# Side jobs of 18 attention slots dealt out anew between GpSimd, ScalarE, VectorE and TensorE

## The reference

```python
scores = q @ k.T / 8; mask: 0 <= i - j < 64; attn = softmax(scores) @ v
x = attn as (2304, 512)
xn = x / sqrt(mean(x * x) + 1e-6) * rms_g          # by token
x = (silu(xn @ w_gate) * (xn @ w_val)) @ w_out     # d_ff 1536
out = (relu(x @ w_in) ** 2) @ w_out2               # d_ff 2048
```

## Time and profile before

| | |
|---|---|
| median of 3 runs | 885.33 us (883.21 to 885.65) |
| the profiled execution | 885.68 us, span 884.0 us |
| TensorE busy | 858.6 us, 97% |
| VectorE busy | 548.2 us, 62% |
| ScalarE busy | 472.3 us, 53% |
| GpSimd busy | 543.9 us, 62% |
| mean granted TensorE clock | 0.994 |

### The profile page before, as it was taken

One profiled execution on the slowest core, in us unless ns is written; L12 is line 12 of the kernel. 1 busy time (PEld: TensorE's weight loads), 2 busy tenths in 40 slices (PEclk: granted clock), 3 DMA queues, 4 the chain that ended last, 5 costly groups with the idle time before them and its releaser, 6 DMA issues.

```text
span 884.0 us, 16543 instructions
## 1 busy us (share of the span) xinstructions
PE 858.6 (97%) x6388; PEld 846.9 (96%) x6388; DVE 548.2 (62%) x617; ACT 472.3 (53%) x1000; POOL 543.9 (62%) x517
## 2 busy tenths in 40 slices
PE   6787999999999999999999999999999999999998
PEld 5676999999999999999999999999999999999998
DVE  4767766558658548755556777676477675577222
ACT  5996565645565635455555455444455443555332
POOL 3664488674589755378857468563386744585332
PEclk9998999999999999999999999999999999999999
DMA  7863122212222212222212222222422221421222
GB/s 239 282 222 100 42 72 73 66 49 65 86 72 73 63 52 70 70 80 73 73 54 68 76 66 73 66 60 61 150 70 77 61 61 60 150 74 29 54 67 96
DMA packets 87007, 75.01 MB, mean 85 GB/s; under 512 B 5520, under 2 KB 70032, under 8 KB 86928
## 3 DMA queue, kind: packets, MB, share of 16 engines
q1 hardware_dynamic: 86784, 73.65, 27.9%
q10 hardware_dynamic: 144, 0.29, 0.1%
HBM read 69.21 MB, written 4.72 MB: 84 GB/s over the span
## 4 chain that ended last, share of the span: by engine, by line
PE 93%; ACT 2%; DVE 2%; DMA 1%; issue 1%; POOL 1%; SPq 0%; DVEq 0%; POOLq 0%
PE banks L703 30%; PE banks L705 30%; PE banks L704 30%; ACT probs L976 2%; PE banks L613 1%; PE banks L669 1%; DMA q_sb<-in_qT 1%; DVE probsT L1224 1%; PE banks L684 0%; PE banks L677 0%; PE banks L643 0%; POOL sq L507 0%; DVE neg_max L1211 0%; DVE banks L1204 0%; DVE acts L1164 0%
## 5 line engine op out<-in xcount | busy, mean ns | idle before, releaser
L703 PE MATMUL banks<-xc_hi,w_hi 128*128 128x384 f32 x844 | 282.5, 335 | 0.2 <-DVE xc_lo L1196 0.2
L705 PE MATMUL banks<-xc_hi,w_lo 128*128 128x384 f32 x844 | 281.9, 334 | 0.0
L704 PE MATMUL banks<-xc_lo,w_hi 128*128 128x384 f32 x844 | 281.9, 334 | 0.0
L564 POOL TENSOR_TENSOR d_lo<-d_raw,d_hi 128x512 fp32r<-128x512 f32 x84 | 127.3, 1516 | 174.4 <-ACT d_hi L899 174.4
L703 PE MATMUL banks<-hs_hi,d_hi 128*128 128x384 f32 x672 | 225.1, 335 | 0.1
L705 PE MATMUL banks<-hs_hi,d_lo 128*128 128x384 f32 x672 | 224.5, 334 | 0.0
L704 PE MATMUL banks<-hs_lo,d_hi 128*128 128x384 f32 x672 | 224.5, 334 | 0.0
L1302 DVE TENSOR_TENSOR hs_lo<-h,hs_hi 128x768 fp32r<-128x768 f32 x84 | 86.4, 1029 | 137.1 <-ACT hs_hi L899 136.9
L703 PEld LDWEIGHTS banks<-xc_hi,w_hi 128*128 128x128 f32 x844 | 158.5, 188 | 0.5 <-DVE xc_lo L1196 0.5
L704 PEld LDWEIGHTS banks<-xc_lo,w_hi 128*128 128x128 f32 x844 | 158.5, 188 | 0.0
L705 PEld LDWEIGHTS banks<-xc_hi,w_lo 128*128 128x128 f32 x844 | 158.4, 188 | 0.0
(11 more groups left out here) (87 smaller groups left out, 1072.9 us busy)
## 6 DMA issues: line engine op xcount, KB each, us to landing
d_raw<-in_w_down SPq DMA_DIRECT2D x48, 256.0 KB, 2.6
w_raw<-in_w_gate SPq DMA_DIRECT2D x36, 256.0 KB, 2.9
w_raw<-in_w_val SPq DMA_DIRECT2D x72, 128.0 KB, 2.8
d_raw<-in_w_out SPq DMA_DIRECT2D x36, 256.0 KB, 2.6
v_sb<-in_v_rows SPq DMA_DIRECT2D x16, 384.0 KB, 3.8
w_raw<-in_w_in SPq DMA_DIRECT2D x24, 256.0 KB, 2.7
w_raw<-in_w_in SPq DMA_DIRECT2D x48, 128.0 KB, 2.6
q_sb<-in_qT SPq DMA_DIRECT2D x16, 288.0 KB, 4.8
```

The lines of the kernel that those rows point to most:

```text
L564: nc.gpsimd.tensor_tensor(d_lo[m % 2][:], d_raw[m % 2][:], d_hi[m % 2][:].bitcast(F32), ALU.subtract).then_inc(dlo_done, 1)
L703: pe.matmul(ps, w_h, v_h, start=first, stop=False, skip_group_check=joined)
L704: pe.matmul(ps, w_h, v_l, start=False, stop=False, skip_group_check=joined)
L705: return pe.matmul(ps, w_l, v_h, start=False, stop=last, skip_group_check=joined)
```

## The change

Round 0 gets its squares in part from GpSimd: all four of the first half (slots 8 and 9), two of four of the second (slot 11; the other two stay on ScalarE). GpSimd no longer sums the four pieces: PE does, with `first_sums`, 12 one-column products that add up in PSUM after slot 10, and 12 more after slot 12. The high parts of the first two weight tiles go from ScalarE to GpSimd (slots 5, 7 and 10), the second tile's low parts from slots 7 and 8 to 14 and 15. Root, inverse, diagonals, both spreads, normalisations and high and low parts of the tokens come one slot earlier, and the second spread goes into bank 5, after slot 16, where it waits for the normalisations of the first half. The plain products of the first tile begin in slot 17. v has four buffers, and its loads are issued behind those of k and q. Six products of the identity with itself come ahead of the first scores.

```diff
--- before.py
+++ after.py
@@
-VR = 3
+VR = 4
+WARM = 6
@@ sync: the loads of the attention stage
             for i in range(SEQS):
-                if i + 1 < SEQS:
-                    load_v(i + 1)
                 if i + QR < SEQS:
                     load_k(i + QR)
                     load_q(i + QR)
+                if i + 1 < SEQS:
+                    load_v(i + 1)
@@ gpsimd
-            def add_squares(c, k):
...
+            def high1_plain(u):
+                pool.wait_ge(w_raw_in[u], 32)
+                nc.gpsimd.tensor_copy(w_hi[u][:, 0:3 * HALF_K], raw_part(u, RAW_A21, 3)).then_inc(hi1_done, 1)
+
+            def high2_plain(u):
+                pool.wait_ge(w_a22_in[u], 16)
+                nc.gpsimd.tensor_copy(w_hi[u][:, P_A22 * HALF_K:(P_A22 + 1) * HALF_K],
+                                      raw_part(u, RAW_A22)).then_inc(hi2_done, 1)
+
+            def square_half(k, c):
+                of = half_cols(0, k, c)
+                nc.gpsimd.tensor_tensor(squares[0][k][:, c * NT:(c + 1) * NT], of, of, ALU.mult).then_inc(sq_pool, 1)
@@ gpsimd, after the scaling of slot g
-                if g in (5, 7):
-                    low1_plain((g - 5) // 2)
-                if g in (6, 8):
-                    low2_plain((g - 6) // 2)
-                if g in (9, 10, 11):
-                    add_squares(0, g - 8)
-                if g == 12:
-                    for k in (1, 2, 3):
-                        add_squares(1, k)
+                if g == 5:
+                    high1_plain(0)
+                if g == 6:
+                    low1_plain(0)
+                if g == 7:
+                    high2_plain(0)
+                    low2_plain(0)
+                if g in (8, 9):
+                    pool.wait_ge(o_out, O_DONE[A_GROUP + 1])
+                    for k in (2 * (g - 8), 2 * (g - 8) + 1):
+                        square_half(k, 0)
+                if g == 10:
+                    high1_plain(1)
+                    high2_plain(1)
+                if g == 11:
+                    pool.wait_ge(o_out, O_DONE[B_GROUP + 1])
+                    square_half(0, 1)
+                    square_half(1, 1)
+                if g == 13:
+                    diagonals(0)
                 if g == 14:
-                    diagonals(0)
+                    low1_plain(1)
+                if g == 15:
+                    low2_plain(1)
@@ tensor, slot 0
                         pe.wait_ge(consts, 6)
+                        for n in range(WARM):
+                            pe.matmul(bank[5][:, 0:P], ident[:], ident[:], start=True, stop=True)
                         pe.wait_ge(first_in, 32)
@@ tensor
+            def first_sums(c, ps):
+
+                for n in range(c * TB // 2, (c + 1) * TB // 2):
+                    for k in range(KT):
+                        mm = pe.matmul(ps[:, n:n + 1], squares[0][k][:, n * P:(n + 1) * P], ones[:, 0:1],
+                                       start=k == 0, stop=k == KT - 1)
+                if c == 1:
+                    mm.then_inc(ms_mm, 1)
@@ tensor, the slots
             for g in range(TAIL):
-                if g == 17:
-                    pe.wait_ge(exp_done, 17)
-                    spread_half(1, bank[1])
                 slot(g)
-                if g == 13:
-                    token_sums(0, bank[5])
-                if g == 15:
-                    spread_half(0, bank[5])
-                if g == 18:
+                if g == 10:
+                    pe.wait_ge(consts, CONSTS)
+                    pe.wait_ge(sq_pool, KT)
+                    first_sums(0, bank[5])
+                if g == 12:
+                    pe.wait_ge(sq_pool, KT + 2)
+                    pe.wait_ge(sq_done, 2)
+                    first_sums(1, bank[5])
+                if g == 14:
+                    spread_half(0, bank[5])
+                if g == 16:
+                    pe.wait_ge(norm_done, KT)
+                    spread_half(1, bank[5])
+                if g == 17:
+                    pe.wait_ge(exp_done, 17)
                     pe.wait_ge(lo1_done, 1)
                     plain(0, "ga", P_A11, "B11")
...
@@ scalar, the slots
-                if g in (4, 6):
-                    high1((g - 4) // 2)
-                if g in (5, 7):
-                    high2((g - 5) // 2)
-                if g == A_GROUP + O_LAG:
-                    act.wait_ge(o_out, O_DONE[A_GROUP + 1])
-                if 0 <= g - A_GROUP - O_LAG < KT:
-                    square_half(g - A_GROUP - O_LAG, 0)
                 if g == B_GROUP + O_LAG:
                     act.wait_ge(o_out, O_DONE[B_GROUP + 1])
-                    for k in range(KT):
-                        square_half(k, 1)
-                if g == 13:
+                    square_half(2, 1)
+                    square_half(3, 1)
+                if g == 12:
                     root(0)
-                if g in (16, 17):
-                    x_high(0, ("B11", "B21")[g - 16], KT)
-                if g in (18, 19):
-                    x_high(0, ("B12", "B22")[g - 18], 2 * KT)
+                if g in (15, 16):
+                    x_high(0, ("B11", "B21")[g - 15], KT)
+                if g in (17, 18):
+                    x_high(0, ("B12", "B22")[g - 17], 2 * KT)
```

More of the change, by code:

```diff
@@ L671, in token_sums @@
             def token_sums(q, ps):
-                pe.wait_ge(sq_sum, 3 * q + 6)
-                if q == 0:
-                    pe.wait_ge(consts, CONSTS)
+                pe.wait_ge(sq_sum, 3 * q)
                 for n in range(TB):
-                    mm = pe.matmul(ps[:, n:n + 1], diag[min(q, 1)][:, n * P:(n + 1) * P], ones[:, 0:1],
+                    mm = pe.matmul(ps[:, n:n + 1], diag[1][:, n * P:(n + 1) * P], ones[:, 0:1],
                                    start=True, stop=True)
                 mm.then_inc(ms_mm, 1)
+            def first_sums(c, ps):
[5 more added lines that the diff above has]
+                    mm.then_inc(ms_mm, 1)
             def spread_part(q, ps, n):
@@ L743, in _ @@
                     plain(0, "vb", P_A21, "B12")
+                if g == 20:
                     pe.wait_ge(x_split, split_count(0, "B22"))
@@ L901, in high1 @@
             def high1(u):
-                if u < PLAIN:
-                    act.wait_ge(w_raw_in[u % 2], 32)
-                    copy(w_hi[u % 2][:, 0:3 * HALF_K], raw_part(u, RAW_A21, 3), hi1_done)
-                    return
                 act.wait_ge(s_add, 4 * steps_done(u - 1) + 3)
@@ L915, in high2 @@
             def high2(u):
-                if u < PLAIN:
-                    act.wait_ge(w_a22_in[u % 2], 16)
-                    copy(w_hi[u % 2][:, P_A22 * HALF_K:(P_A22 + 1) * HALF_K], raw_part(u, RAW_A22), hi2_done)
-                    return
                 act.wait_ge(s_add, 4 * steps_done(u))
@@ L1228, in _ @@
                         ALU.mult).then_inc(pt_out, 1)
+                if g == 12:
+                    mean_square(0, bank[5])
                 if g == 13:
-                    mean_square(0, bank[5])
-                if g == 14:
                     inverse(0)
-                if g in (15, 16):
-                    if g == 15:
+                if g in (14, 15):
+                    if g == 14:
                         dve.wait_ge(rb_first, 1)
                         dve.wait_ge(gain_in, 16)
-                    for k in (2 * (g - 15), 2 * (g - 15) + 1):
+                    for k in (2 * (g - 14), 2 * (g - 14) + 1):
                         normalise(half_cols(0, k, 0), k, bank[5][:, 0:NT])
-                if g in (17, 18):
-                    if g == 17:
+                if g in (16, 17):
+                    if g == 16:
                         x_low(0, "B11")
                         dve.wait_ge(rb_first, 2)
-                    for k in (2 * (g - 17), 2 * (g - 17) + 1):
-                        normalise(half_cols(0, k, 1), k, bank[1][:, 0:NT])
+                    for k in (2 * (g - 16), 2 * (g - 16) + 1):
+                        normalise(half_cols(0, k, 1), k, bank[5][:, 0:NT])
+                if g == 17:
+                    x_low(0, "B21")
                 if g == 18:
-                    x_low(0, "B21")
-                if g == 19:
                     x_low(0, "B12")
                     x_sum(0, "T3")
-                if g == 20:
+                if g == 19:
                     x_low(0, "B22")
```

18 lines of the change are left out of this document (6 added, 12 removed).

## The result

| | before | after |
|---|---|---|
| median | 885.40 us (882.53 to 887.25, 20 runs) | 882.87 us (879.40 to 885.08, 20 runs) |
| the profiled execution | 885.68 us, span 884.0 | 882.57 us, span 880.8 |
| mean granted TensorE clock | 0.994 | 0.994 |

The ratio is 0.9973, with a 95% interval of 0.9961 to 0.9984: faster by 2.5 us. I had forecast 5.2: the time lies in the range, but only half of the gain came.

The account below looks back on a forecast made before the run. TensorE works unbroken from 85.59 us, so only reaching that stretch earlier counts. Stretch gains 0.4 + 1.25 - 0.5 - 0.45 + 3.9 + 1.55 = 6.15, less 0.95 for stalls, leave 5.2 us: 880.1 us, range 876.8 to 884.5.

Parts of the forecast that it names:

- Slots 12 to 16: Stretch between exponentials of slots 12 and 16: 16.69 us before, 17.15 after, a loss of 0.45, sums mostly hidden.
- Rival 3: Lower clock comes in slots 13 to 16, one slot of it costing 2.7 us: 882.8 us, chance 0.08.
- slots 0 to 5: Stretch from slot 0 to 5: 18.06 us before, 17.65 after, as a weight's high part leaves ScalarE; gain 0.4.
- the tail: After slot 17, to PE's full stretch: 6.81 us before, 5.25 after, with work moved one slot ahead; gain 1.55.
- the 0.95 us set aside for stalls: Subtracted from the summed gain of 6.15 us for PE stalls on nothing visible, expected to return in part.
- Slots 10 to 12: Stretch with PE's first block of sums, 2.9 us: 8.47 us before, 9.0 after, a loss of 0.5.
- rival 2: PE's sums take a full record each, 6.0 us in place of 2.9: 884.1 us, chance 0.13.
- Slots 5 to 10: Waits for q and k vanish, loop and GpSimd work come next: 18.27 us before, 17.0 after; gain 1.25.
- Slot 16 to 17: Second spread no longer waits for slot 16's exponentials: 8.40 us before, about 4.5 after; gain 3.9.
- Squares and casts: On GpSimd in slots 5 to 11: 1.0 us per 128x384 square, 0.9 per 128x768 cast.
- Rival 1: GpSimd becomes the bound in slots 5 to 14, its work meeting the doubled rate: 890.6 us, chance 0.07.
- Rival 4: Clock rises earlier: 0.9 us in the first scores, 0.3 in slots 1 to 3; 878.9 us, chance 0.12.

Follow-up runs that it names:

- run with 64 columns: Changed kernel with each of TensorE's sums of squares 64 columns wide in place of one: 881.56 us, ratio 0.9973.
- table early: Changed kernel with one small exponential right behind the root, so the table load doesn't wait for the output copy: 882.73 us, ratio 0.9968.
- the run with 64 columns alone: Kernel before with only the second spread moved and the sums on PE, these 64 columns wide in place of one: 882.29 us, ratio 0.9975.

## Why the prediction was off

**What bounds the kernel: right.** The stretch behind the slots is filled as before (796.95 of 799.99 us busy), and the result is found ahead of it.

**The failed step is "Slots 12 to 16", in the words "all but that lies beside slot 12 or below the table loads. Periods of 6.3 and 3.3".** The 6.3 was 9.02. I had followed two paths, scores to exponentials and root to table load, and let the sums hide below the second. The path that ends last is a third: sums, scores, value product, ScalarE's copy of the outputs, table load, exponentials. The load is not cover for PE's work but stands behind it, as ScalarE makes its copy first. From the rows, at full clock and with 2.9 us of sums, this chain would come to some 6.9 us: 0.6 more than forecast. It is an estimate: sums end near 56.4, scores 1.1, value product 1.2, copy 0.7, load 1.3. The run with 64 columns agrees (8.06 less its stall of 1.18 is 6.9), and the one profile at full clock in which the sums began earlier took 6.33, the 6.3 of the forecast. So the order of ScalarE is worth 0 to 0.6 us, and the other 2.1 us are the lower clock from 55.4 us on, in the sums, the scores and the value product. The sum of the prediction has PE at full clock there and puts nothing for it. The runs bear out the two together (both removed: period 5.98, time 2.3 to 2.8 us lower) and the chain (table early: the copy no longer ahead of the load). The split between clock and order rests on rows, and on one soft comparison across sessions.

**The rival of the lower clock came nearest, in part by luck.** Rival 3 had it in slots 13 to 16 for one slot and gave 882.8 us, with a chance of 0.08. That this is the measured 882.87 almost to the digit is luck: it charges 2.7 us for the clock where the rows give 2.1, and the rest is the chain and the 0.8 us of slots 0 to 5, less what the tail gained beyond its forecast and the 0.95 us set aside for stalls. Its reason did not hold either: a clock that falls after PE has stood waiting. Here PE had waited only 0.78 us (and 0.79 in the run with 64 columns, where the clock stayed up); what PE was doing when the clock fell were one-column products, which the earlier trace rows and the profile of before (low clock from 58.7 to 62.1 us, right behind `token_sums`) already showed once. I made four times as many of these products and did not ask what they had done to the clock. The Trainium skill, TensorE: Matmul & The Clock Gate, Part 1, which I had cited for the warm-up, says that activity brings the clock up. The trace agrees in so far as the six products had it up by slot 0 or 1 in five of eight profiles and in none without them; the sums show a second side, a PE that is busy in the records and yet loses its clock.

**The first part of the sums, "Slots 10 to 12", was right:** 9.06 against 9.0, block 2.74 against 2.9 (so rival 2, at 6.0, falls). In three other profiles the clock fell there as well, with 6.27, 6.72 and 6.77 for the period that took 5.43 here, and in a fourth it was low already, with 9.65: that the forecast held in this one is luck.

**Slots 5 to 10: right in the waits, wrong in what comes next.** The q waits fell from 3.5 to 0.7 us, and the stretch came out 0.4 us short of its forecast. "What is late next is the loop itself" was too simple: by the run with the loads alone their worth in time is zero, 2.9 us of waits giving 2.9 us of stalls. The allowance of 0.95 us for stalls was meant for this and was too small by that run; in the changed kernel the stalls were 3.2 us. Only the run with the loads of before speaks for some worth of the loads there, 1.1 to 2.6 us. In slots 0 to 5, a stall of 1.74 us and the lower clock behind it made 18.43 us of the 17.65 forecast.

**Slot 16 to 17 and the tail: right.** 4.61 for 4.5, and 2.4 for 1.55. The spread alone, at 879.72 us, brings more than the whole change. The tail's gain comes from the work moved one slot ahead: the tail is 802.8 to 803.1 us in the profiles of the change and of five kernels made from it (804.0 in two more, in which the clock fell once more at 79 and 85 us), and 804.8 to 805.2 in all those with that work where it was.

**Squares and casts: right in sign.** 0.80 us for a square in place of 1.0, 0.82 for the cast in place of 0.9. Rival 1 (GpSimd at half rate, 890.6 us) never showed: the six squares took 0.80 to 0.83 us each.

**Rival 4** (clock up earlier) did not hold in this profile, where the first scores kept their 2.00 us. In others the clock was up by slot 0 or 1 and low again in slot 3, and the run without the warm-up puts its worth at about 1 us, not clear of nothing.

## What to carry to other kernels

Before work is moved below a long instruction of another engine, write down that engine's own order: what stands between the cover and the next batch, and whether that in turn waits for the work being moved. Before work of a kind is multiplied, look in the profile at the clock behind the instances that are there already. A transfer wait that is taken away in a loop full of small waits should be tried alone, as it may come back under another name. When a change of several parts gains little, run its strongest part alone: here it gained about twice what the whole did.

## What the chip showed that I had not expected

**The clock falls behind blocks of one-column products.** Of 13 blocks of 24 records with one column that began at full clock (seven profiles), 10 had the clock fall during the block or within 4.1 us of its start. Shorter blocks: 4 of 6 with 12 records, none of 2 with 6. Blocks of the same count with 64 columns: none of 5; a sixth began when the clock was already low. The stationary blocks are the same and the time is the same, 2.74 us and 2.79 us, so the wider products cost nothing. This is a pattern over profiles, not proof of a mechanism. The clock fell at other places too, with no sums near (between 21 and 36 us in nine of the 17 profiles); some of these falls came at the end of a stall of PE (of 1.74 us at 24.8 in the change, of 2.17 us at 48.9 in the run with 64 columns alone), and what causes them these runs don't show.

**Fewer waits for transfers did not mean less time.** Before, the waits for q and the stalls with no releaser were 3.5 and 2.9 us; with the new loads alone 0.6 and 5.8, the same sum. That is no rule: in the changed kernel they were 0.7 and 3.2, in the changed kernel without the warm-up 0.8 and 7.0, with the casts and the new loads 0.8 and 3.7, and this last kernel was yet 2 us slower than with the old loads (3.0 and 4.1). The profile lists instruction fetches on a queue of their own, but no run moved them, so that these stalls are fetches is only a guess.

**A square is cheaper on GpSimd than a sum of two buffers,** 0.80 us against 1.00 us for 128x384. Both have two operands; in the square they are the same one, and the sum writes over one of its own. Which of the two matters was not tried.
